# Dense queries, per-head level matmuls and a moved recurrence in an attention kernel with two MLP layers

## The reference

```python
# q, k, v, alpha: (4, 8, 768, 48); tokens N = 3072, model width 384
for t in range(S):
    state = alpha[:, :, t, :, None] * state + np.einsum('bhd,bhe->bhde', k[:, :, t], v[:, :, t])
    y[:, :, t] = np.einsum('bhd,bhde->bhe', q[:, :, t], state)
# x: y as (3072, 384)
h = x @ w_in                                        # 384 x 2048
g = np.where(h > 0.0, h, np.exp(np.minimum(h, 0.0)) - 1.0)
x = g @ w_out
p = domain_probs / (domain_probs.sum(-1, keepdims=True) + 1e-09)
for e in range(4):
    h = np.maximum(x @ w1[e], 0.0)                  # 384 x 1024
    out += p[:, e:e + 1] * (h @ w2[e])
```

## Time and profile before

| | |
|---|---|
| median of 3 runs | 1472.08 us (1470.0 to 1472.56) |
| the profiled execution | 1472.1 us, span 1470.3 us |
| mean granted TensorE clock | 0.982 |
| busy: PE, PEld | 1370.7 us (93%), 1144.0 us (78%) |
| busy: DVE, ACT, POOL | 940.2 us (64%), 664.6 us (45%), 582.1 us (40%) |

### The profile page before, as it was taken

How to read it: one execution, slowest core, us unless ns; L and a number is a source line. 1 busy time by engine, 2 the same in 40 slices (tenths; PEclk the granted TensorE clock), 3 DMA queues, 4 the chain that set the end, 5 groups by cost and what they waited for, 6 DMA issues and landing times.

```text
span 1470.3 us, 19162 instructions
## 1 busy us (share of the span) xinstructions
PE 1370.7 (93%) x6632; PEld 1144.0 (78%) x6632; DVE 940.2 (64%) x1238; ACT 664.6 (45%) x1171; POOL 582.1 (40%) x544
## 2 busy tenths in 40 slices
PE   1479999999999999989999989999999999999998
PEld 1468788887778888778888778888777888887886
DVE  6767757548857746866745885755784774554443
ACT  1256644435653434653443563443565343464331
POOL 7664264218526314717411935521752631100012
PEclk9689999999999999999999999999999999999999
DMA  6043253443343252434253434344324323243330
GB/s 233 21 145 108 80 173 93 128 137 113 88 154 115 79 180 75 137 86 169 82 168 102 125 89 171 90 120 148 109 93 158 113 80 89 87 147 97 97 98 32
DMA packets 89906, 169.41 MB, mean 115 GB/s; under 512 B 34897, under 2 KB 36689, under 8 KB 89809
## 3 DMA queue, kind: packets, MB, share of 16 engines
q1 hardware_dynamic: 89808, 168.17, 36.5%
HBM read 161.79 MB, written 6.34 MB: 114 GB/s over the span
## 4 chain that ended last, share of the span: by engine, by line
PE 46%; issue 27%; DVE 16%; ACT 6%; POOL 3%; DMA 1%; SPq 0%; DVEq 0%; POOLq 0%; ACTq 0%
PE ps_h L416 7%; PE ps_h L417 7%; PE ps_h L418 7%; PE ps_o L416 6%; PE ps_o L418 6%; PE ps_o L417 6%; DVE w_lo L583 6%; DVE elu_out L595 3%; PE ps_att L365 3%; ACT g_hi L785 2%; DVE scores L526 2%; DVE q_level L568 2%; POOL acc L917 2%; PE ps_att L397 2%; DVE q_low L513 1%
## 5 line engine op out<-in xcount | busy, mean ns | idle before, releaser
L416 PE MATMUL ps_h<-x_hi,w_lo 128*128 128x512 f32 x864 | 342.0, 396 | 24.5 <-DVE elu_out L595 11.2
L416 PE MATMUL ps_o<-g_hi,w_lo 128*128 128x512 f32 x864 | 347.7, 402 | 6.0 <-DVE g_lo L599 6.0
L583 DVE TENSOR_TENSOR w_lo<-w_stage,w_hi 128x768 fp32r<-128x768 f32 x288 | 326.8, 1136 | 35.1 <-ACT w_hi L763 30.0
L417 PE MATMUL ps_h<-x_lo,w_hi 128*128 128x512 f32 x864 | 339.2, 393 | 0.0
L418 PE MATMUL ps_h<-x_hi,w_hi 128*128 128x512 f32 x864 | 339.2, 393 | 0.0
L418 PE MATMUL ps_o<-g_hi,w_hi 128*128 128x512 f32 x864 | 337.4, 390 | 0.0
L417 PE MATMUL ps_o<-g_lo,w_hi 128*128 128x512 f32 x864 | 336.7, 390 | 0.0
L790 ACT ACTIVATE g_hi<-ps_h 128x512 fp32r<-128x512 f32 x192 | 114.8, 598 | 484.3 <-PE ps_h L418 483.8
L603 DVE SCALAR_TENSOR_TENSOR g_lo<-ps_h,g_hi 128x512 fp32r<-128x512 f32 x192 | 132.5, 690 | 277.6 <-ACT g_hi L790 277.4
L219 POOL TENSOR_TENSOR products<-q_block,k_block 128x384 f32<-128x384 f32 x165 | 193.5, 1183 | 123.4 <-DVE scores L526 116.1
L763 ACT CAST w_hi<-w_stage 128x768 fp32r<-128x768 f32 x288 | 239.2, 832 | 1.7
(11 more groups left out here) (59 smaller groups left out, 1297.0 us busy)
## 6 DMA issues: line engine op xcount, KB each, us to landing
w_stage<-in_w SPq DMA_DIRECT2D x288, 384.0 KB, 3.1
v_tok<-in_v SPq DMA_DIRECT2D x12, 576.0 KB, 4.6
alpha<-in_a SPq DMA_DIRECT2D x12, 512.0 KB, 6.7
k_level<-in_k SPq DMA_DIRECT2D x12, 512.0 KB, 7.5
q_low<-in_q SPq DMA_DIRECT2D x12, 512.0 KB, 8.2
p_rows<-p_norm SPq DMA_DIRECT2D x6, 1024.0 KB, 8.7
out<-acc SPq DMA_DIRECT2D x18, 256.0 KB, 4.1
q_block<-in_q_blocks SPq DMA_DIRECT2D x11, 384.0 KB, 3.9
```

What stands on the lines that cost most here:

```text
L416: nc.tensor.matmul(dst, lhs[1], rhs[0], start=first, stop=False)
L417: nc.tensor.matmul(dst, lhs[0], rhs[1], start=False, stop=False)
L583: nc.vector.tensor_tensor(wl[n % WRING][:], stage[n % STAGE][:], wh[n % WRING][:].bitcast(F32), ALU.subtract).then_inc(w_low, 1)
```

## The change

- The queries stay dense in `QL`, now two buffers of the plain layout, loaded by DMA directly. `QT`, `QD`, `expand` and `left` are gone, and the clearing of the slots with them.
- A level piece on PE is 8 logical matmuls, one per head, each over 64 rows (0 to 63 or 64 to 127) and 64 query columns. Head 0 of each pair writes to one PSUM bank, head 1 to another. Every level piece uses the same two banks and waits for the rectangles of the piece before it. The banks of K, KV and Y are fixed.
- `rectangles` copies from the two banks: 8, 4 and 2 copies for levels 4, 5 and 6, each of 4 heads, for 4, 2 and 1 of 8 heads. DVE's `pairs` is one operation over 128 rows for two over 64.
- The order in the main loop: the pieces of the first unit stand at j = 16 to 27 (were 8 to 19), those of the second at 28 to 39 as before. Low queries, keys and totals of the second unit go to j = 14 to 20 (were 20 to 26), its block operations to 18 to 31; block operations are spread over 14 steps for 12. The DMAs of a unit move to j = 8 and 29 and those of v to 2 and 30 (for 15 and 35, 21 and 41). ACT does the piece of step J at the end of its pass J, DVE and GpSimd in pass J + 1; at j = 15 ACT and DVE make the second MLP's input and its first two ReLU rows before the weights of step J + 4.

```diff
-EXPAND = FIRST - 3
 LEAD = 2
+PARTS = 14
+LOW_AT, BLOCK_AT, PE_AT = (0, 14), (0, 18), (16, 28)
...
+def block_part(i):
+
+    return [n for n in range(NOPS) if n * PARTS // NOPS == i]
+
+
+def events_of_slot(o):
 
     u, i = divmod(o, SLOTS)
-    if i < FIRST:
-        return None
-    kind, c, l = PIECES[i - FIRST]
-    return kind, 2 * u + c, l, NPE * u + i - FIRST
+    events = [("low", u, i)] if i < LEVELS else []
+    if u == 0 and i <= PARTS:
+        events += [("block", 0, i), ("block", 1, i)]
+    return events + ([("piece", u, i - FIRST)] if i >= FIRST else [])
+
+
+def events_of_step(J):
+
+    t, j = divmod(J, STEPS)
+    events = []
+    if t < TILES - 1 and J >= 0:
+        for v in range(2):
+            u = 2 * t + 2 + v
+            for kind, at, count in (("low", LOW_AT, LEVELS), ("block", BLOCK_AT, PARTS + 1), ("piece", PE_AT, NPE)):
+                if 0 <= j - at[v] < count:
+                    events.append((kind, u, j - at[v]))
+    return events
+
+
+def piece(u, i):
+    kind, c, l = PIECES[i]
+    return kind, 2 * u + c, l
...
-def pieces_of_step(J):
-    t, j = divmod(J, STEPS)
-    return [LEAD * SLOTS + 2 * SLOTS * t + j] if t < TILES - 1 and j < 2 * SLOTS else []
...
-        QT = sb("q_low", [P, PAIRS, UNIT])
-        QL = sb("q_level", [P, PAIRS, 2, UNIT])
+        QL = sbs("q_level", 2, [P, PAIRS, UNIT])
...
-        QD = sbs("q_dense", 2, [P, PAIRS, P])
...
+        level_banks = [ps_a[sd][:, 0:PAIRS * HALF] for sd in range(2)]
+
+        def bank_of(kind, c):
+            return ps_a[{("K", 0): 2, ("K", 1): 0, ("KV", 0): 1, ("Y", 0): 2, ("Y", 1): 0, ("KV", 1): 1}[kind, c]]
...
-                if u >= 1:
-                    sp.wait_ge(q_slots, u)
-                sp.dma_start(QT[:], q_d[u]).then_inc(q_in, 16)
+                if u >= 2:
+                    sp.wait_ge(y_done, 2 * (u - 1))
+                sp.dma_start(QL[s][:], q_d[u]).then_inc(q_in[s], 16)
...
-                    if u < UNITS and j == SLOTS * v + FIRST + 6:
+                    if u < UNITS and j == BLOCK_AT[v] + PARTS + 2:
                         place_scores(u)
-                    if u + 1 < UNITS and j == SLOTS * v + FIRST + 7:
+                    if u + 1 < UNITS and j == BLOCK_AT[v] + PARTS + 1:
                         load_blocks(u + 1)
+                    if u + 1 < UNITS and j == (8, 29)[v]:
                         load_unit(u + 1)
-                    if u + 1 < UNITS and j == SLOTS * v + SLOTS + 1:
+                    if u + 1 < UNITS and j == (2, 30)[v]:
...
+            def pairs(g, l):
+                u, s, c = g // 2, g // 2 % 2, g % 2
                 h = 1 << l
                 if l == LOW:
-                    pe.wait_ge(q_slots, u + 1)
+                    pe.wait_ge(q_low, LOW * (u + 1))
                     pe.wait_ge(k_low, LOW * (u + 1))
+                    if u:
+                        pe.wait_ge(xa_ready, 2 * u)
+                        pe.wait_ge(st_ready, 2 * u + 1)
                 else:
                     pe.wait_ge(q_up, lev(g, l - 1))
                     pe.wait_ge(k_up, lev(g, l - 1))
-                t = slice(P * (g % 2), P * (g % 2 + 1))
+                if lev(g, l) > 1:
+                    pe.wait_ge(rect, lev(g, l) - 1)
+                t = slice(P * c, P * (c + 1))
                 for pr in range(PAIRS):
-                    mov = QL[:, pr, :, t].rearrange("p s (m two h) -> p s m two h", two=2, h=h)[:, :, :, 1, :]
-                    last = nc.tensor.matmul(bank(n)[:, pr * P:(pr + 1) * P], KL[s][:, pr, t], mov, start=True, stop=True)
+                    for sd in range(2):
+                        r, dst = slice(HALF * sd, HALF * (sd + 1)), level_banks[sd][:, HALF * pr:HALF * (pr + 1)]
+                        right = QL[s][r, pr, t].rearrange("p (m two h) -> p m two h", two=2, h=h)[:, :, 1, :]
+                        last = nc.tensor.matmul(dst, KL[s][r, pr, t], right, start=True, stop=True)
                 last.then_inc(step_done, 1)
 
-            def transpose_k(o, g):
...
+                if g % 2:
+                    pe.wait_ge(rect, lev(g, LEVELS - 1))
+                elif g:
+                    pe.wait_ge(xa_ready, g - 1)
...
+            def outer(g):
                 s = g // 2 % 2
+                if g % 2:
+                    pe.wait_ge(st_ready, g + 1)
+                else:
+                    pe.wait_ge(rect, lev(g + 1, LEVELS - 1))
...
-                    nc.tensor.matmul(dst, ST[g % 3][:, pr, :], QD[g % 2][:, pr, :], start=True, stop=False)
+                    dst = bank_of("Y", g % 2)[0:2 * D, pr * P:(pr + 1) * P]
+                    nc.tensor.matmul(dst, ST[g % 3][:, pr, :], QL[s][:, pr, P * (g % 2):P * (g % 2 + 1)], start=True, stop=False)
...
-                if l == LEVELS - 1 and g >= 2:
-                    dve.wait_ge(y_done, g - 1)
-
-                def right(a):
-                    return a.rearrange("p a (m two h) -> p a m two h", two=2, h=h)[:, :, :, 1, :]
-                for sd in range(2):
-                    r = slice(HALF * sd, HALF * (sd + 1))
-                    old = right(QL[r, :, sd, t])
-                    new = right(QD[g % 2][r]) if l == LEVELS - 1 else old
-                    last = nc.vector.tensor_tensor(new, old, decays(l, s, g, 0)[r].broadcast_to([HALF, PAIRS, HALF // h, h]), ALU.mult)
-                last.then_inc(q_up, 1)
+                right = chunk(QL, g).rearrange("p a (m two h) -> p a m two h", two=2, h=h)[:, :, :, 1, :]
+                nc.vector.tensor_tensor(right, right, decays(l, s, g, 0).broadcast_to([P, PAIRS, HALF // h, h]), ALU.mult).then_inc(q_up, 1)
...
-                for o in pieces_of_step(J - 1) if J else []:
-                    attention(o)
-                if J + SPLIT < ALL:
-                    lower_w(J + SPLIT)
                 if j == N1 - 1:
                     lower_x2(t)
                     lower_relu(J + 1)
                     lower_relu(J + 2)
+                for event in events_of_step(J - 1):
+                    attention(*event)
+                if J + SPLIT < ALL:
+                    lower_w(J + SPLIT)
...
-            def expand(u):
-                act.wait_ge(q_low, LOW * (u + 1))
-                if u:
-                    act.wait_ge(q_up, lev(2 * u - 1, LEVELS - 1))
-                    act.wait_ge(q_left, 2 * u)
-                else:
-                    act.wait_ge(q_clear, 1)
-                for sd in range(2):
-                    r = slice(HALF * sd, HALF * (sd + 1))
-                    last = nc.scalar.copy(QL[r, :, sd, :], QT[r])
-                last.then_inc(q_slots, 1)
-
-            def left(g):
-                act.wait_ge(q_up, lev(g, LEVELS - 2))
-                if g >= 2:
-                    act.wait_ge(y_done, g - 1)
-                for sd in range(2):
-                    r = slice(HALF * sd, HALF * (sd + 1))
-                    last = nc.scalar.copy(QD[g % 2][r, :, 0:HALF], QL[r, :, sd, P * (g % 2):P * (g % 2) + HALF])
-                last.then_inc(q_left, 1)
...
-                src = bank_of("L", g, l)[:].rearrange("p (a t) -> p a t", t=HALF)
-                for m in range(HALF // h):
-                    last = nc.scalar.copy(PW[g % 2][2 * m * h:(2 * m + 1) * h, :, (2 * m + 1) * h:(2 * m + 2) * h],
-                                          src[2 * m * h:(2 * m + 1) * h, :, m * h:(m + 1) * h])
+                for sd in range(2):
+                    src = level_banks[sd].rearrange("p (a t) -> p a t", t=HALF)
+                    dst = PW[g % 2][:].rearrange("p (a two) t -> p a two t", two=2)[:, :, sd, :]
+                    for m in range(HALF // h):
+                        last = nc.scalar.copy(dst[2 * m * h:(2 * m + 1) * h, :, (2 * m + 1) * h:(2 * m + 2) * h],
+                                              src[2 * m * h:(2 * m + 1) * h, :, m * h:(m + 1) * h])
...
-                for o in pieces_of_step(J - 1) if J else []:
-                    attention(o)
-                if J + SPLIT < ALL:
-                    high_w(J + SPLIT)
                 if j == N1 - 1:
                     high_x2(t)
                     high_relu(J + 1)
                     high_relu(J + 2)
+                if J + SPLIT < ALL:
+                    high_w(J + SPLIT)
                 for n in hidden_of_step(J):
                     if is_elu(n):
                         exponent(n)
                     else:
                         high_relu(n)
+                for event in events_of_step(J):
+                    attention(*event)
```

More of the change, by code:

```diff
@@ L486, in _, with attention @@
         def _(dve):
-            def attention(o):
-                u, i = divmod(o, SLOTS)
-                if i < LOW:
+            def attention(kind, u, i):
+                if kind == "low" and i < LOW:
                     low_queries(u, i)
-                if u > 1:
+                elif kind == "block" and u == 0:
+                    for n in block_part(i):
+                        early_block(n)
+                elif kind == "block":
```

(20 more changed lines are left out.)

151 lines of the change are left out of this document (56 added, 95 removed).

## The result

The changed kernel takes 1482.51 us in the median of 4 runs (1480.93 to 1483.27), the kernel before 1472.07 (1470.0 to 1472.56) beside it: ratio 1.0069, 95% interval 1.0054 to 1.0085. It is slower by 10.4 us, where 1448.7 was forecast. In the profiled executions the spans are 1480.7 and 1470.3 us, so these two traces carry the whole difference.

The account below looks back on a forecast made before the run. PE was taken to bound almost all of the main loop, DVE and the chain of dependences the lead-in. Stalls -34.4, level matmuls +9.0 and lead-in +2 took 1472.1 to 1448.7 us, range 1438 to 1499.

Parts of the forecast that it names:

- term 2: ELU steps and reset of the main loop: stalls go once pieces leave, 34.4 us saved, bounds 20 and 45.
- Term 1: Level matmuls on PE: each of 60 main-loop pieces goes from 0.90 to 1.05 us, +9 us; +54 at 1.80.
- rival (a): Level pieces on PE: loads go one after another, 1.80 us per piece, 1496.7 us in all; chance 0.36.
- the side-by-side case: Level pieces on PE: two heads work in parallel, 1.05 us per piece with issue as floor; chance 0.44.
- rival (b): Level pieces on PE: partial overlap or a cost per full/half-row change, about 1.4 us per piece, 1470.7 us; chance 0.14.
- the 0.99 at j = 7: PE's wait for elu_out in tile 1, laid to ACT's expansion of the queries, said to go.
- the two of 0.69: PE's waits for a level piece's operands in tile 1, laid to DVE's updates and reductions, said to go.
- the bound of 20: Low bound of the stall saving, 20 us, if block products over 14 instead of 12 steps keep DVE late.
- The three early stalls: Stalls at j = 3 to 5, 0.9 us each, from low-query products on DVE beside busy GpSimd; 2.7 us stay.
- Term 3: Work on ACT, DVE, GpSimd and SP in ReLU steps, claimed to hide behind PE and costed at nothing.
- Term 4: Lead-in: single buffer unhidden, savings on DVE and expansion; about +2 us at 1.05 per piece, bounds -4 and +8.
- (c): ELU steps: DVE still late, stalls give back 20 instead of 34.4 us, heads side by side, 1463 us; chance 0.06.

Follow-up runs that it names:

- level_twice: The changed kernel with the 8 logical matmuls of each level piece issued twice in a row; 1547.91 us in one run.
- old_full: old_order with level pieces of 4 matmuls over all 128 rows, mixing two heads' scores; 1448.17 us, ratio 0.9848.
- old_order: The changed kernel with pieces, low queries, block operations and DMAs back at their old steps, block operations over 12; 1467.96 us, ratio 0.9979.
- pieces_moved: old_order with only the first unit's twelve pieces moved to j = 16 to 27, as in the change; 1473.2 us, ratio 1.0015.
- old_passes: old_order with ACT's and DVE's order within a pass as before: recurrence event ahead of ELU and ReLU operations, x2 last; 1480.85 us, ratio 1.0068.

## Why the prediction was wrong

By the terms of its sum, in us of the span (the measured term 2 is the remainder from above):

| term | forecast | measured |
|---|---|---|
| 1, 60 level pieces | +9 | +22.2 |
| 2, stalls | -34.4 | -18.6 |
| 4, lead-in | +2 | +6.8 |
| sum | -23.4 | +10.4 |

**Term 1: right mechanism, one cost left out.** The two heads do work side by side, as the forecast assumed and rival (a) denied: loads in pairs, 0.111 per pair, nothing for 16 matmuls more than the 0.89 of eight full passes (level_twice). Issue set no floor either: 0.89 is below my 0.96. The failing step is "I take 1.05 for the side-by-side case": it priced issue, which costs nothing, and left the change of form to rival (b). (One of its readings was off as well: it set 243 ns for 96-column matmuls against 275 for 128, but 243 is the shortest of the first, whose median is 275 too; the sum did not use it.) The piece is 0.89 + 0.38 = 1.27, the step 5.35, between the 5.1 of the forecast and the 5.5 of (b), whose second reason, a cost at each change, is what happened. The Trainium skill ("TensorEngine Tiling (Array Packing)", Key Properties) says that tiles work in parallel and that a change of mode drains the array. The runs agree with both, and put 0.34 to 0.38 us on the second, as far as it is the rows and not the columns that count; the prediction quoted it without a term in its sum.

**Term 2: the step that decided.** Its size was not far off: in old_full, without either fault, the main loop is 27.4 us shorter than before, and its 60 pieces of 0.93 cost 1.8 more, so 29 of the 34.4 came back. (That its time is also the forecast is in part chance: pieces that cost 1.8 where 9 were forecast, and a lead-in 3.9 longer where 2 were, even out the missing 5.) What it said of two waits held: the 0.99 at j = 7, laid to ACT's expansion, and the two of 0.69 are gone in old_order too, whose pieces have not moved. But the rest of the step tied the gain to the moved pieces, and three of its statements failed. That the pieces' leaving empties the reset: old_order, with the pieces there, has 14.77, pieces_moved 15.85. By what is left, the load that held x_lo back was DVE's and ACT's work of the padded form, and the change takes that away wherever the pieces stand. That the reset's one level piece "stands ahead of hidden row 18 and covers most of that": it does stand there, which is at 415.88, behind all three waits (405.10, 409.10 and 411.61), and covers none; in the changed kernel 16.78 - 13.51 = 3.3 us stay, where I had left 0.6:

```profile
409.10 0.50 PE L433 MATMUL ps_o<-g_hi,w_lo 128*128 128x512 f32 x1 [1.64 <-DVE g_lo L608]
...
411.61 0.47 PE L433 MATMUL ps_h<-x_hi,w_lo 128*128 128x512 f32 x1 [0.16 <-DVE x_lo L618]
...
415.88 1.11 PE L375 MATMUL ps_att<-q_level,k_level 64*128 64x64 f32 x16
```

That 14 steps instead of 12 are harmless: the bound of 20 named this very risk; it costs 6.8 us of the main loop and takes the term from about 25 to 18.6, below the bound. The three early stalls stayed, as said; one of them grew.

**Term 3** costed ACT, DVE and GpSimd at nothing and was right for the order that the change chose. old_passes shows how narrow that was: its placement of ACT's copies hides 13 us. DVE's update, taken at 865 ns, is 849 in the median of the changed kernel and 425 in old_order.

**Term 4: right sign and reason, too small.** I worked with pieces of 1.05. In this stretch the granted clock is 0.50, that is 1.2 GHz, after 5.29 us in which PE waited; the windows of the changed kernel and of the kernel before:

```profile
76.29:95.14 18.85, 11.77 (x96) 10.86 (x96) 2.13 (x5) 5.94 (x26) 3.85 (x5) 0.50 0.41 146
```

```profile
79.64:88.16 8.52, 8.20 (x48) 7.73 (x48) 5.69 (x10) 4.91 (x16) 3.84 (x5) 0.74 0.65 236
```

A piece lasts 1.97 us there, and the waits between them add 1.90, 1.89, 1.24, 1.24 and 0.81: 18.9 us in place of the 14 forecast, against 3.4 gained by an earlier start.

**The rivals.** (b)'s cost and (c)'s stalls came true together: 1472.1 + 22.2 - 18.6 + 6.8 = 1482.5. Each was weighed alone (1470.7 and 1463), both faster than before; their sum with the longer lead-in is slower. The sign that I expected from serial loads came from smaller losses at once.

## What to carry to other kernels

Before work is moved off a busy place, ask what waits it covers: short matmuls between a producer and its reader are cover, and to move them can cost more than they take. In this kernel a matmul form over half the rows was free in itself where the halves alternate, but every change between forms was paid, so put as many such matmuls as possible into one place. And where several rivals are independent costs rather than alternatives, add them before reading off the sign.

## What was unexpected of the hardware

- A change from matmuls over 128 rows and 512 columns to ones over 64 rows and 64 columns and back costs 0.34 to 0.38 us at a granted clock of 1.00, the same for 16 and for 32 matmuls between. The first half-row load starts only 0.31 us after the start of the last wide matmul, where a full-row one starts with it.
- Two row halves load and multiply side by side when they alternate (0.111 us per pair of passes). With eight of one half ahead of the other the piece is 0.50 us longer.
- DVE's g_lo, 0.69 us alone, lasts the rest of a running GpSimd product of the recurrence plus some 0.55 when it starts beside one (0.88 to go: 1.42; 1.09 to go: 1.64). No run took the product away alone.
- After a wait of 2.7 us in old_passes the next step of PE ran at a granted clock of 0.75 in tiles 2 to 4, and at 1.00 in tile 1 after the same wait.
